# Attention and two-stage expert kernel: routing rounds, splits and first loads at other places

## The chip, the cores and the metric

The kernel runs on one core of a Trainium2 chip. The metric is the device time of one execution, in microseconds (us); lower is better. Names of engines: PE is TensorE (matmuls; PEld its weight loads), DVE is VectorE, ACT is ScalarE, POOL is GpSimd, and SP is SyncE, which here only issues DMAs.

## What is computed

```
# attention, 4 batches x 8 heads x 576 positions x 64
scores = q @ k.T / 8 + alibi bias, causal, window of 128; x = softmax(scores) @ v      -> x: 2304 x 512
# routing: every token gets one of 8 experts, 288 tokens each
logits = x @ w_gate                      # 2304 x 8
for idx in argsort(-logits.flatten()):   # greedy, best score first, until an expert is full
    tok, e = idx // 8, idx % 8; assign if tok is free and expert e has fewer than 288
for e in range(8):  y[mask_e] = relu(x[mask_e] @ w1[e]) @ w2[e]        # 512 -> 1024 -> 512
# dense layer
h = y @ w_in; out = (h * sigmoid(h)) @ w_out                            # 512 -> 2048 -> 512
```

## The kernel before

All work is written out by hand for each engine; semaphores order it, and every engine executes its list in order. There are two blocks.

**Attention.** 16 groups (batch, pair of heads) are worked through in 65 slots; group g's five row tiles (four of 128 rows, one of 64) are finished one after the other. When a group's tiles are normalised (DVE, `normalise`, L705), PE turns them (`turn_x`: four tiles into one PSUM bank, L410, the fifth into another, L413), DVE copies the first four to `xT` (`copy_x`, L626), ACT the fifth (`copy_x_end`, L551), and PE multiplies with the gate weights (`gate_logits`, L422, five matmuls, ten in the trace). For the last group nothing is left to run beside this.

**Routing of an expert.** The next expert to be filled, and its 288 tokens, are found by rounds of a search for a threshold. A round has an even part (PE counts, 20 small matmuls, L1102; DVE compares, `reached`, L1381) and an odd part (PE sums, L1106; DVE finds the digit and writes the next comparison matrix `test`). For expert 0, which is found before any expert runs, DVE writes `test` in two halves of 10 tiles (L1353, L1356), and PE counts the first (L1094) while DVE makes the second (L1102). For experts 1 to 7 it is one instruction (L1360). After the rounds come three closing parts: one in which the ranks are summed (L1109; before it the expert's number goes to SP, which may then load weights), one in which token numbers are collected (L1115; DVE then writes `tokens`, on which POOL's gather waits, and after some bookkeeping `out_tokens`), and one that updates the counts of free places (L1120, which waits for `out_tokens`). Expert j > 0 has 13 parts, numbered 0 to 12: rounds 0 to 9, ranks 10, tokens 11, counts 12. Expert 0 has 15.

**Experts.** Expert i is an A stage (expert i's two matrices, 16 slots) and an M stage (the dense layer for its batch, 32 slots): 48 slots in all. A slot is either `a` (12 matmuls into an `hp` bank; there are two) or `b` (12 matmuls in A, 6 or 9 in M, into `acc`). The order is a0, a1, a2, b0, a3, b1, a4, b2 and so on, so that b(f) runs two `a` slots behind a(f). Behind an M `a` slot ACT takes the sigmoid (`gate`, L1307), DVE multiplies (`h_raw`, L1561), ACT rounds (`h_h`, L1315) and POOL takes the rest (`h_l`, L1078). PE's a(f+2) reuses the bank of a(f) and so waits for `h_raw` of a(f), and b(f) waits for `h_l` of a(f).

All operands are split into a rounded and a remaining part. For a weight tile ACT makes the high part (L1256 for w1, L1261 for w2), DVE the low part of w1 (`low_a`, L1498), POOL that of w2 (`low_b`, L1064). Rings of four hold the tiles of each. For w of a new expert's first four tiles the splits stand at slots given by SPLIT_A and SPLIT_B, the loads in the order LOADS on SP's queue.

The parts of expert j's routing run inside expert j-1's 48 slots, at slots given by HOOK_LIST, after a set-up (SETUP_AT: `setup`, L1366 to the first `test`, some 15 DVE instructions). At a slot, the part comes ahead of the slot's own work, on PE as on DVE. The gather for expert j (`fetch`, three indirect DMAs of 96 rows, L1042) stands on POOL at the slot of part 11, and PE turns the gathered rows at slot 45 (X_AT).

For expert 0, SP issues eight weight loads (w1 and w2 tiles 0 to 3, alternating) as soon as the expert is known; POOL issues the gather a little later, then runs `low_b` for four tiles, while DVE waits for the gather to be issued (`fetch_sent`) and then runs `low_a`.

## Time and profile before

| | us |
|---|---|
| median of 3 runs | 894.79 |
| lowest and highest | 894.15, 895.1 |
| the profiled execution's own time | 896.79 |
| its span in the trace | 895.0 |
| PE busy | 846.1 (95%) |
| DVE, ACT, POOL busy | 503.9, 344.8, 290.1 |
| mean granted clock of PE | 0.975 |

The span is from the first to the last instruction; about 1.8 us lie around it. PE's busy time is modelled from pipelined matmuls, so small waits of PE can be hidden in it. In the text, a row `241.75 0.50 PE` means: begins 241.75 us after the span's start and takes 0.50 us.

### The profile page before, as it was taken

To read this page: it belongs to the slowest core of one execution; us is meant where nothing else is said; L and a number is where in the kernel's file an instruction comes from. 1 tells how busy PE (TensorE), PEld (TensorE's weight loads), DVE (VectorE), ACT (ScalarE), POOL (GpSimd) and SP (SyncE) were. 2 spreads that over 40 slices of the span, in tenths; PEclk is the share of its full clock that TensorE was granted. 3 is DMA by queue.
4 is the path that set the end of the run, shared out by engine and by line. 5 is a ranking of instruction groups with operands and counts; after the bars stand their busy time and mean duration, and the time that the engine had idled before them with its cause. 6 is when DMAs were issued, how large, how long until landed. Compare 5 with 4: busy or idle time off the path is not lost.

```text
span 895.0 us, 17483 instructions
## 1 busy us (share of the span) xinstructions
PE 846.1 (95%) x6605; PEld 790.2 (88%) x6605; DVE 503.9 (56%) x1618; ACT 344.8 (39%) x814; POOL 290.1 (32%) x306
## 2 busy tenths in 40 slices
PE   6999999962999999999999999999999999999998
PEld 6999999951998998899899889998998899899996
DVE  6667676757667386466628462666376466632111
ACT  4666666621333432433333233333332433433222
POOL 1333233413124422622432244225322522532223
PEclk9999999965899999999999999999999999999999
DMA  6666666414203121230412040403121240312000
GB/s 154 168 153 158 152 154 156 112 28 121 83 13 121 44 76 37 86 107 13 122 44 76 1 121 1 123 9 122 54 65 55 68 114 5 121 60 61 1 1 35
DMA packets 117252, 71.42 MB, mean 80 GB/s; under 512 B 61616, under 2 KB 103600, under 8 KB 117168
## 3 DMA queue, kind: packets, MB, share of 16 engines
q1 hardware_dynamic: 114192, 60.85, 25.2%
q0 software_dynamic: 2976, 9.44, 3.4%
q8 instruction: 53, 0.87, 0.4%
q14 instruction: 31, 0.25, 0.1%
HBM read 60.83 MB, written 9.44 MB: 79 GB/s over the span
## 4 chain that ended last, share of the span: by engine, by line
PE 65%; DVE 10%; DMA 2%; issue 1%; ACT 1%; POOL 1%; SPq 0%; POOLq 0%; DVEq 0%
PE hp L1148 11%; PE hp L1150 10%; PE hp L1149 10%; PE acc L1218 7%; PE acc L1220 7%; PE acc L1219 7%; PE acc L1148 4%; PE acc L1150 3%; PE acc L1149 3%; PE rt L1102 2%; DVE test L1360 2%; DVE h_raw L1561 1%; DMA rows<-x_rows,tokens 1%; DVE wa_l L1498 1%; DMA wa_raw<-in_moe_w_dram 1%
## 5 line engine op out<-in xcount | busy, mean ns | idle before, releaser
L1078 POOL TENSOR_TENSOR h_l<-h_raw,h_h 128x256 fp32r<-128x256 f32 (+1 forms) x128 | 103.6, 809 | 268.2 <-ACT h_h L1315 268.0
L1148 PE MATMUL hp<-xy_h,res_h 128*128 128x256 f32 (+1 forms) x512 | 154.6, 302 | 2.3 <-DVE h_raw L1561 2.3
L1561 DVE TENSOR_TENSOR h_raw<-hp,gate 128x256 f32<-128x256 f32 (+1 forms) x128 | 58.3, 456 | 171.1 <-ACT gate L1307 170.1
L1149 PE MATMUL hp<-xy_l,res_h 128*128 128x256 f32 (+1 forms) x512 | 151.4, 296 | 0.0
L1150 PE MATMUL hp<-xy_h,res_l 128*128 128x256 f32 (+1 forms) x512 | 151.3, 295 | 0.0
L1064 POOL TENSOR_TENSOR wb_l<-wb_raw,wb_h 128x512 fp32r<-128x512 f32 x64 | 86.5, 1353 | 139.6 <-ACT wb_h L1261 139.4
L1307 ACT ACTIVATE gate<-hp 128x256 f32<-128x256 f32 (+1 forms) x128 | 52.4, 409 | 171.0 <-PE hp L1150 170.0
L1218 PE MATMUL acc<-res_h,h_h 128*128 128x512 f32 x288 | 116.7, 405 | 0.0
L1220 PE MATMUL acc<-res_h,h_l 128*128 128x512 f32 x288 | 113.6, 395 | 0.0
L1219 PE MATMUL acc<-res_l,h_h 128*128 128x512 f32 x288 | 113.5, 394 | 0.0
L1148 PEld LDWEIGHTS hp<-xy_h,res_h 128*128 128x128 f32 x512 | 96.6, 189 | 8.5 <-DVE h_raw L1561 4.9
L1149 PEld LDWEIGHTS hp<-xy_l,res_h 128*128 128x128 f32 x512 | 96.4, 188 | 3.5
L1150 PEld LDWEIGHTS hp<-xy_h,res_l 128*128 128x128 f32 x512 | 96.5, 188 | 0.0
L1315 ACT ACTIVATE h_h<-h_raw 128x256 fp32r<-128x256 f32 (+1 forms) x128 | 56.9, 445 | 101.1 <-DVE h_raw L1561 101.1
L1148 PE MATMUL hp<-xy_h,wa_h 128*128 128x288 f32 x256 | 77.9, 304 | 0.6 <-DVE xy_l L1505 0.6
L1498 DVE TENSOR_TENSOR wa_l<-wa_raw,wa_h 128x512 fp32r<-128x512 f32 x64 | 60.3, 944 | 30.8 <-ACT wa_h L1256 26.8
L1149 PE MATMUL hp<-xy_l,wa_h 128*128 128x288 f32 x256 | 76.5, 299 | 0.0
L1150 PE MATMUL hp<-xy_h,wa_l 128*128 128x288 f32 x256 | 76.4, 299 | 0.0
L1148 PE MATMUL acc<-h_h,wb_h 128*128 128x288 f32 x256 | 76.3, 298 | 0.0
L1150 PE MATMUL acc<-h_h,wb_l 128*128 128x288 f32 x256 | 75.2, 294 | 0.0
L1149 PE MATMUL acc<-h_l,wb_h 128*128 128x288 f32 x256 | 75.2, 294 | 0.0
L480 PE MATMUL o_ps<-v_rows,pT 128*128 128x65 f32 x576 | 71.4, 269 | 0.0
(214 smaller groups left out, 1754.3 us busy)
## 6 DMA issues: line engine op xcount, KB each, us to landing
wa_raw<-in_moe_w_dram SPq DMA_DIRECT2D x64, 256.0 KB, 2.9
wb_raw<-in_moe_w_dram SPq DMA_DIRECT2D x64, 256.0 KB, 3.1
q_rows<-in_q_dram SPq DMA_DIRECT2D x32, 128.0 KB, 3.8
k_rows<-in_k_dram SPq DMA_DIRECT2D x32, 128.0 KB, 3.0
v_rows<-in_v_dram SPq DMA_DIRECT2D x32, 128.0 KB, 2.4
stage<-in_moe_w_in_dram SPq DMA_DIRECT2D x8, 512.0 KB, 4.5
x_rows<-x_rows_sb SPq DMA_DIRECT2D x16, 256.0 KB, 4.2
stage<-in_moe_w_out_dram SPq DMA_DIRECT2D x8, 512.0 KB, 4.6
```

Source lines behind the costliest of these rows:

```text
L480: last = nc.tensor.matmul(o_ps[s % 2][:, o:o + D + 1], weights, v_rows[g % RING_IN][:, kt, h, :], start=(i == 0), stop=(i == len(blocks) - 1))
L1064: pool.tensor_tensor(wb_l[w % RING][:], wb_raw[w % RING][:], wb_h[w % RING][:].bitcast(FP32), ALU.subtract).then_inc(wb_low, 1)
L1078: pool.tensor_tensor(h_l[:, cols], h_raw[:, cols], h_h[:, cols].bitcast(FP32), ALU.subtract).then_inc(g_low, 1)
L1148: nc.tensor.matmul(out_, weights_h, cols_h, start=start, stop=False)
L1149: nc.tensor.matmul(out_, weights_h, cols_l, start=False, stop=False)
L1150: return nc.tensor.matmul(out_, weights_l, cols_h, start=False, stop=stop)
L1218: nc.tensor.matmul(acc[t][:], h_h[:, m], res_h[:, o:o + DM], start=(b == 0), stop=False)
L1219: nc.tensor.matmul(acc[t][:], h_h[:, m], res_l[:, o:o + DM], start=False, stop=False)
L1220: last = nc.tensor.matmul(acc[t][:], h_l[:, m], res_h[:, o:o + DM], start=False, stop=(b == FT2 - 1))
L1315: nc.scalar.activation(h_h[:, h_cols(s, f)], h_raw[:, h_cols(s, f)], ACT.Copy).then_inc(g_high, 1)
L1498: nc.vector.tensor_tensor(wa_l[w % RING][:], wa_raw[w % RING][:], wa_h[w % RING][:].bitcast(FP32), ALU.subtract).then_inc(wa_low, 1)
L1561: nc.vector.tensor_tensor(h_raw[:, h_cols(s, f)], hp[(A_NO[s, f] - 1) % 2][:, 0:width], gate[:, 0:width], ALU.mult).then_inc(g_done, 1)
```

## The change

Five things are moved, and no arithmetic is added or taken away.

1. **Attention end.** For the last group, `turn_x` is cut in two: three tiles are turned ahead of the last weighted values (they are normalised by then), two behind them. Their logits are computed in the same two pieces. The copy of the three tiles goes from DVE to ACT (`copy_x_last`).
2. **Rounds of expert 0.** `test` is written as 14 and 6 tiles instead of 10 and 10.
3. **Slots of the parts** (counted in expert j-1's 48 slots):

| | set-up | parts 0 to 12 |
|---|---|---|
| before | 3 | 8, 9, 12, 13, 16, 17, 21, 22, 24, 25, 28, 31, 33 |
| after, j = 1 | 5 | 9, 10, 12, 13, 16, 20, 24, 25, 28, 29, 32, 35, 39 |
| after, j > 1 | 3 | 8, 9, 12, 13, 16, 20, 24, 25, 28, 29, 32, 35, 39 |

The loads of the next expert, which wait for part 9, go with it from slot 25 to 29, the gather with part 11 from 31 to 35.

4. **Splits of an expert's first four tiles** go from slots 31, 33, 35, 37 (`b` slots) to 38, 40, 42, 44 (`a` slots).
5. **First weights of expert 0.** SP issues w1 tiles 0 and 1, then waits until the gather is issued (`fetch_sent`), then w2 tile 0, w1 tile 2 and the rest. The splits of w2's four tiles and of w1's tile 3 go into the first slots of the A stage.

```diff
+SETUP_AT = {FIRST[2 * _j - 2] + (5 if _j == 1 else 3): _j for _j in range(1, E)}
+HOOK_LIST = {_j: [FIRST[2 * _j - 2] + _n for _n in ((9, 10, 12, 13) if _j == 1 else (8, 9, 12, 13))
+                  + (16, 20, 24, 25, 28, 29, 32, 35, 39)] for _j in range(1, E)}
...
+AHEAD = 14
+SECOND = 672
...
+LOADS = [("a", 0), ("a", 1), ("b", 0), ("a", 2), ("b", 1), ("a", 3), ("b", 2), ("b", 3)] + LOADS
+SPLIT_A, SPLIT_B = {0: [3]}, {0: [0], 1: [1], AT[0, "b", 0]: [2], AT[0, "b", 1]: [3]}
...
-        _n = max(FIRST[_s - 1] + 13, HOOK_LIST[_w // FT1][CLOSE[_w // FT1] - 1] + 6) + 2 * _f
+        _n = max(FIRST[_s - 1] + 13, HOOK_LIST[_w // FT1][CLOSE[_w // FT1] - 1] + 9) + 2 * _f
...
+                if (kind, w) == LOADS[2]:
+                    sp.wait_ge(fetch_sent, 1)
...
             fetch(0)
             pool.memset(mark[:], 0.0).then_inc(fetch_sent, 1)
-            for w in range(RING):
-                low_b(w)
...
-            for w in range(RING):
-                high_a(w)
-                high_b(w)
+            high_a(0)
+            high_a(1)
             for c in range(DC):
                 high_x(0, c, acc[c])
+            high_a(2)
...
+            turn_x_main(NG - 1)
             weighted_values(NS - 1)
-            turn_x(NG - 1)
-            gate_logits(NG - 1)
+            bank("e", NG - 1)
+            gate_logits(NG - 1, slice(0, main_tiles(NG - 1)))
+            turn_x_end(NG - 1)
+            gate_logits(NG - 1, slice(main_tiles(NG - 1), TB))
...
+            def copy_x_last(g):
+
+                n = TURN_NO["x", g]
+                w = P * main_tiles(g)
+                act.wait_ge(turned, n + 1)
+                act.wait_ge(lg_done, g)
+                nc.scalar.activation(xT[:, 0:w], m_ps[n % 2][:, 0:w], ACT.Copy).then_inc(x_taken, 1)
```

What this moves, as the engines' own lists show it. First PE at the end of attention (o_ps are the weighted values, m_ps<-x_rows_sb the turned tiles, m_ps<-wg,xT the logits); before:

```order
L458 MATMUL t_ps<-ident,p_even 128x2x64 x2
L480 MATMUL o_ps<-v_rows,pT 128x65 x8
L410 MATMUL m_ps<-ident,x_rows_sb 128x128 x4
L413 MATMUL m_ps<-ident,x_rows_sb 128x128
L422 MATMUL m_ps<-wg,xT 128x8 x5
```

And the same place on PE after the change:

```order
L479 MATMUL t_ps<-ident,p_even 128x2x64 x2
L501 MATMUL o_ps<-v_rows,pT 128x65 x4
L421 MATMUL m_ps<-ident,x_rows_sb 128x128 x3
L501 MATMUL o_ps<-v_rows,pT 128x65 x4
L442 MATMUL m_ps<-wg,xT 128x8 x3
L430 MATMUL m_ps<-ident,x_rows_sb 128x128 x2
L442 MATMUL m_ps<-wg,xT 128x8 x2
```

Three turned tiles and their logits now stand ahead of or beside the last values; two tiles and two logit matmuls are left behind them.

Next ACT at the start of the experts (wa_h and wb_h are high parts of w1 and w2 tiles, xy_h of the gathered rows, h_h the first results of the A stage); before:

```order
L1256 ACTIVATE wa_h<-wa_raw_3793 128x512
L1261 ACTIVATE wb_h<-wb_raw_3797 128x512
L1256 ACTIVATE wa_h<-wa_raw_3794 128x512
L1261 ACTIVATE wb_h<-wb_raw_3798 128x512
L1256 ACTIVATE wa_h<-wa_raw_3795 128x512
L1261 ACTIVATE wb_h<-wb_raw_3799 128x512
L1256 ACTIVATE wa_h<-wa_raw_3796 128x512
L1261 ACTIVATE wb_h<-wb_raw_3800 128x512
L1266 ACTIVATE xy_h<-acc 128x288 x4
L1301 ACTIVATE h_h<-hp 128x288 x2
```

The same place on ACT after the change:

```order
L1297 ACTIVATE wa_h<-wa_raw_3811 128x512
L1297 ACTIVATE wa_h<-wa_raw_3812 128x512
L1307 ACTIVATE xy_h<-acc 128x288 x4
L1297 ACTIVATE wa_h<-wa_raw_3813 128x512
L1342 ACTIVATE h_h<-hp 128x288
L1297 ACTIVATE wa_h<-wa_raw_3814 128x512
L1302 ACTIVATE wb_h<-wb_raw_3815 128x512
L1342 ACTIVATE h_h<-hp 128x288
L1297 ACTIVATE wa_h<-wa_raw_3811 128x512
L1302 ACTIVATE wb_h<-wb_raw_3816 128x512
```

Two weight tiles instead of eight stand ahead of the gathered rows; the others come behind the first results.

Last DVE in expert 0's M stage, between parts 11 and 12 of expert 1's routing (out_tokens ends part 11, spare is part 12, h_raw is an `a` slot's work, wa_l a split); before:

```order
L1479 TENSOR_TENSOR chosen<-chosen,tmp 128x20
L1463 SCALAR_TENSOR_TENSOR out_tokens<-rt,idx_low 32x1
L1463 SCALAR_TENSOR_TENSOR out_tokens<-rt,idx_low 32x2 x4
L1498 TENSOR_TENSOR wa_l<-wa_raw_3793,wa_h 128x512
L1561 TENSOR_TENSOR h_raw<-hp,gate 128x256
L1486 TENSOR_TENSOR spare<-spare,rt 128x8
L1487 TENSOR_SCALAR full<-spare 128x8
```

The same place on DVE after the change:

```order
L1518 TENSOR_TENSOR chosen<-chosen,tmp 128x20
L1502 SCALAR_TENSOR_TENSOR out_tokens<-rt,idx_low 32x1
L1502 SCALAR_TENSOR_TENSOR out_tokens<-rt,idx_low 32x2 x4
L1599 TENSOR_TENSOR h_raw<-hp,gate 128x256 x2
L1537 TENSOR_TENSOR wa_l<-wa_raw_3811,wa_h 128x512
L1525 TENSOR_TENSOR spare<-spare,rt 128x8
L1526 TENSOR_SCALAR full<-spare 128x8
```

Two `a` slots instead of one lie between the two parts, and the first split stands behind them.

## Rows read from the trace of the kernel before

**Rows 1.** The page: the granted TensorE clock in 40 slices, in tenths.

```profile
PEclk9999999965899999999999999999999999999999
```

**Rows 2.** Waits of PE, whole span: line, what ended them, us, times, longest.

```profile
PE acc L1235 <- DMA rows<-x_rows,tokens: 8.5, 1, 8.5
PE rt L1120 <- DVE out_tokens L1463: 8.1, 7, 1.3
...
PE hp L1148 <- DVE h_raw L1561: 2.3, 6, 0.4
```

**Rows 3.** Timeline, end of attention: start, us, engine, line, operation, [idle before].

```profile
186.97 0.28 DVE L705 TENSOR_TENSOR x_rows_sb<-o_ps,rden 64x128 f32<-64x128 f32 x1
...
187.40 0.92 PE L410 MATMUL m_ps<-ident,x_rows_sb 128*128 128x128 f32 x4 [0.86 <-DVE x_rows_sb L705]
...
188.57 0.28 ACT L551 ACTIVATE xT<-m_ps 128x128 f32<-128x128 f32 x1 [3.35 <-PE m_ps L413]
...
189.14 2.27 PE L422 MATMUL m_ps<-wg,xT 128*128 128x8 f32 x10 [0.61 <-DVE xT L626]
191.45 0.19 DVE L637 TENSOR_TENSOR logits<-m_ps,logits 128x32 f32<-128x32 f32 x1 [2.41 <-PE m_ps L422]
```

**Rows 4.** Timeline, one round of expert 0, DVE and PE.

```profile
198.70 0.65 DVE L1353 SCALAR_TENSOR_TENSOR test<-rungs,base,key_hi 128x410 bf16<-128x410 f32 x1
...
199.41 0.43 PE L1094 MATMUL rt<-choice,test 128*128 128x8 bf16 x10 [1.14 <-DVE test L1353]
199.96 0.43 PE L1102 MATMUL rt<-choice,test 128*128 128x8 bf16 x10
```

**Rows 5.** Timeline, from expert 0's first load to its first product.

```profile
212.15 0.41 SPq L998 DMA_DIRECT2D wa_raw<-in_moe_w_dram  x1
...
218.39 0.92 POOL L1042 DMA_INDIRECT rows<-x_rows,tokens  x1 [0.30 <-issue]
...
219.43 4.80 DVE L1498 TENSOR_TENSOR wa_l<-wa_raw,wa_h 128x512 fp32r<-128x512 f32 x2 [2.32 <-POOL mark L1068]
...
223.25 2.47 PE L1235 MATMUL acc<-ident,rows 96*128 96x96 f32 x12 [8.54 <-DMA rows<-x_rows,tokens]
...
226.33 0.58 PE L1148 MATMUL hp<-xy_h,wa_h 128*128 128x288 f32 x1 [0.60 <-DVE xy_l L1505]
```

**Rows 6.** All 24 gather DMAs (L1042): time from issue to landing.

```profile
DMA to landing us min/median/max: 3.0/3.1/6.0
```

**Rows 7.** Two stretches: busy PE, PEld, DVE, ACT, POOL, granted clock, DMA.

```profile
226.00:232.00 6.00, 5.67 (x24) 5.70 (x25) 3.41 (x11) 1.01 (x3) 0.00 (x0) 0.50 0.14 42
232.00:238.00 6.00, 6.00 (x47) 6.00 (x47) 4.65 (x15) 2.91 (x6) 0.00 (x0) 1.00 0.48 136
```

**Rows 8.** Timeline, parts 11 and 12 of expert 1, in expert 0's M stage.

```profile
279.96 0.66 PE L1115 MATMUL rt<-early,test 128*128 128x18 bf16 x20
...
283.91 0.80 DVE L1463 SCALAR_TENSOR_TENSOR out_tokens<-rt,idx_low 32x1 int32<-32x1 f32 x5
...
284.86 0.17 PE L1120 MATMUL rt<-row_counts,ones 128*128 128x8 bf16 x1 [1.32 <-DVE out_tokens L1463]
```

**Rows 9.** Timeline, part 5 of expert 1, and the PE wait behind it.

```profile
260.13 2.11 DVE L1360 SCALAR_TENSOR_TENSOR test<-rungs,base,key 128x1820 bf16<-128x1820 f32 x1
...
262.63 0.39 PE L1148 MATMUL hp<-xy_h,res_h 128*128 128x256 f32 x1 [0.38 <-DVE h_raw L1561]
```

**Rows 10.** Line L1360, the comparison matrices of experts 1 to 7: duration in ns.

```profile
L1360 DVE SCALAR_TENSOR_TENSOR test<-rungs,base,key_hi x21: 2114/3036/3041, 237.1 to 743.1; 128x1820 bf16<-128x1820 f32 x21
```

**Rows 11.** Timeline, DVE: the set-up of expert 1's routing begins.

```profile
234.72 0.32 DVE L1367 TENSOR_TENSOR liked<-logits,penalty 128x160 f32<-128x160 f32 x1
```

**Rows 12.** The chain that ended last: part 0 of expert 1 (start, us, what).

```profile
241.75 0.50 PE rt L1102 x20
```

**Rows 13.** Timeline, end of expert 0's M stage: its last h_l, and b15.

```profile
303.57 0.74 POOL L1078 TENSOR_TENSOR h_l<-h_raw,h_h 128x256 fp32r<-128x256 f32 x1 [2.10 <-ACT h_h L1315]
...
305.82 0.40 PE L1218 MATMUL acc<-res_h,h_h 128*128 128x512 f32 x1
```

More of the change, by code:

```diff
@@ L141 @@
 RING_NEG = 3
-LG = P
 def slot_units(s):
@@ L596, in _ @@
                     copy_q_low(g + 1)
+            copy_x_last(NG - 1)
             copy_x_end(NG - 1)
@@ L633, in add_logits @@
                     dve.wait_ge(lg_added, g)
-                part = m_ps[TURN_NO["e", g] % 2][:, LG:LG + E * TB].rearrange("p (t e) -> p t e", e=E)
+                o = logits_at(g)
+                part = m_ps[TURN_NO["e", g] % 2][:, o:o + E * TB].rearrange("p (t e) -> p t e", e=E)
                 main = logits[:, TB * b:TB * b + TB - 1, :]
@@ L829, in load_key @@
     return max(AT[s, kind, f], HOOK_LIST[w // FT1][CLOSE[w // FT1] - 1] if w >= FT1 else 0)
-LOADS = sorted([(kind, w) for w in range(E * FT1) for kind in "ab"], key=lambda load: load_key(*load))
-SPLIT_A, SPLIT_B = {}, {}
+LOADS = sorted([(kind, w) for w in range(RING, E * FT1) for kind in "ab"], key=lambda load: load_key(*load))
+LOADS = [("a", 0), ("a", 1), ("b", 0), ("a", 2), ("b", 1), ("a", 3), ("b", 2), ("b", 3)] + LOADS
+SPLIT_A, SPLIT_B = {0: [3]}, {0: [0], 1: [1], AT[0, "b", 0]: [2], AT[0, "b", 1]: [3]}
 for _w in range(RING, E * FT1):
@@ L898, in experts @@
         at_least = test[:, 0:NT * KW[1]].rearrange("p (t k) -> p t k", k=KW[1])
-        halves = [test[:, o:o + KW[0] * NT // 2].rearrange("p (t k) -> p t k", k=KW[0]) for o in (0, SECOND)]
+        pieces = [test[:, o:o + KW[0] * n].rearrange("p (t k) -> p t k", k=KW[0])
+                  for o, n in ((0, AHEAD), (SECOND, NT - AHEAD))]
         onehot = test[:, 0:NT * BLOCK].rearrange("p (t k) -> p t k", k=BLOCK)
@@ L1092, in part @@
                     pe.wait_ge(half_part, h // 2)
-                    for t in range(NT // 2):
+                    for t in range(AHEAD):
                         nc.tensor.matmul(rt[:, 0:E], test[:, KW[0] * t:KW[0] * t + P], choice[:, t, :],
@@ L1098, in part @@
                 if h < CLOSE[j] and h % 2 == 0:
-                    for t in range(NT // 2 if j == 0 and h > 0 else 0, NT):
-                        o = KW[j] * t if j > 0 or h == 0 else SECOND + KW[0] * (t - NT // 2)
+                    for t in range(AHEAD if j == 0 and h > 0 else 0, NT):
+                        o = KW[j] * t if j > 0 or h == 0 else SECOND + KW[0] * (t - AHEAD)
                         last = nc.tensor.matmul(rt[:, 0:E], thresholds[:, o:o + P], choice[:, t, :],
@@ L1351, in try_thresholds @@
                 if j == 0:
-                    t = NT // 2
-                    nc.vector.scalar_tensor_tensor(halves[0], rung[:, None, :].to_broadcast([P, t, k]),
-                                                   base[:, 0:1], keys[:, 0:t, None].to_broadcast([P, t, k]),
-                                                   ALU.add, ALU.is_le).then_inc(half_part, 1)
-                    nc.vector.scalar_tensor_tensor(halves[1], rung[:, None, :].to_broadcast([P, t, k]),
-                                                   base[:, 0:1], keys[:, t:NT, None].to_broadcast([P, t, k]),
-                                                   ALU.add, ALU.is_le).then_inc(dve_part, 1)
+                    for piece, tiles, made in ((pieces[0], slice(0, AHEAD), half_part), (pieces[1], slice(AHEAD, NT), dve_part)):
+                        n = tiles.stop - tiles.start
+                        nc.vector.scalar_tensor_tensor(piece, rung[:, None, :].to_broadcast([P, n, k]), base[:, 0:1],
+                                                       keys[:, tiles, None].to_broadcast([P, n, k]),
+                                                       ALU.add, ALU.is_le).then_inc(made, 1)
                     return
@@ L1539, in _ @@
             low_a(2)
-            low_a(3)
             after(0, HOOKS[0] - 1)
```

51 lines of the change are left out of this document (30 added, 21 removed).

## The prediction

> **What bounds the kernel now.** I read the page first, then the waits of PE, then the timeline at each wait. PE is the bound in attention and in the experts. Between them lies a stretch from about 187 to 226 us in which nothing but expert 0's routing and gather is left, and PE is mostly idle; there the clock granted to PE is down, too [rows 1]. So the time is the length of that stretch plus PE's work, plus the few places where PE waits inside the experts. Those waits are short to list: 8.5 us for expert 0's gathered rows, 8.1 us in seven waits of part 12 for `out_tokens`, 2.3 us in six waits for `h_raw` [rows 2]. The change goes for all three, and for the ends of the stretch.
>
> **Attention end.** Now, from the end of the last normalisation (186.97 + 0.28 = 187.25) to the first added logits at 191.45 are 4.2 us: five turned tiles, two copies, ten logit matmuls at 2.27 / 10, some 0.21 us apart [rows 3]. After the change two tiles, one copy and four matmuls remain. Six matmuls less are 1.3 us. Three turned tiles less are about 0.5 us, since four of them take 0.92 with their latency. The copy on the path is now the one that ends just before 189.14; with 256 columns on ACT it should be near 0.4 (128 columns take 0.28), which gains 0.3. Against that, three turned tiles come ahead of the last weighted values and delay the last normalisation, by 0.4 us, and PE still has the six early logit matmuls beside it, about 0.1 us more. Sum: 1.3 + 0.5 + 0.3 - 0.5 = 1.6 us gained. The ends are 1.2 (more delay ahead) and 2.0 (the clock falls later and the four matmuls run faster). The last rows of x are stored to memory beside this; their DMAs are issued right after the normalisation, so they move back by the same 0.4 us only, and 6 us of ranking lie behind them.
>
> **Rounds of expert 0.** PE counts its first ten tiles 0.71 us after DVE begins the first half, starts on the second ten 1.26 after it, and needs 0.43 for them [rows 4]. DVE's two instructions together have the same length at 14 and 6 tiles. The first takes 4/10 of 0.43 longer, 0.17, so PE starts at 0.88, and 14 matmuls at 0.027 apart ((0.43 - 0.17) / 9, 0.17 being the length of one alone, as in [rows 8]) are issued by 1.26, just when the second part is ready. Then six instead of ten remain: 4 x 0.027 = 0.11 us. Five such rounds: 0.5 us, and not below 0.2.
>
> **Gather of expert 0.** SP's eight loads start at 212.15, ahead of the gather, whose last DMA is issued at 218.39 [rows 5]. The 24 gather DMAs of the kernel land 3.0 to 6.0 us after issue, with a median of 3.1 [rows 6]; expert 0's are the only ones that share the DMA engines with eight fresh weight loads, and PE gets their rows from 223.25 on, turning all twelve pieces in one go. After the change only two loads (0.5 MB) are ahead. They should be in before the first gather moves data, since they lose six rivals. The last gather then lands at 218.39 + 3.1 = 221.5; all pieces of the first two DMAs are turned by then. What follows is one piece (about 0.3), ACT's high part and DVE's low part (0.4 and 0.5) and their hand-overs: first product at about 223.0 against 226.33, so 3.3 us gained. DVE must have `low_a` of tiles 0 and 1 done, which now takes 4.80 us from 219.43 [rows 5] because POOL runs `low_b` at the same time; with `low_b` moved behind, it is over well before 222. Held from both sides: if the loads that now start at 219.4 still disturb the last gather, the gain is 2.3; with nothing left beside it, 3.6. The clock is at its lower level, 1.2 GHz, for the first 5.7 us of products and at 2.4 GHz from 232.0 on [rows 7]. I take it that this stretch moves along unchanged. The late tiles: w1's tile 2 is wanted 5.7 us after the first product (228.7), and is loaded near 223.5; w2's tile 0 one slot, 1.5 us, later. Both have several us in hand, tile 3 and the other w2 tiles about two.
>
> **Part 12.** PE's part 11 ends at 279.96 + 0.66 = 280.6, `out_tokens` at 283.91 + 0.80 = 284.7, and part 12 follows at 284.86; PE has only one `b` and one `a` slot in between, 284.86 - 1.32 - 280.6 = 2.9 us, and waits 1.32 us [rows 8]. So an M slot is 1.4 us. With four slots in between PE has 5.7 us, while DVE's chain stays 4.1 us: the wait goes altogether, in all seven experts. That is 8.1 us [rows 2]. What is late next is `h_raw` of the `a` at slot 36, which DVE begins near 284.8; the `a` at slot 40 wants its bank, five slots behind part 11, at 280.6 + 7.0 = 287.6. So nothing takes the wait's place. POOL issues three gather DMAs there, about 3.5 us during which no `h_l` is made; `b` runs two `a` slots behind, with 5.7 us between a(f) and b(f), so this is covered.
>
> **Part 5.** DVE makes the key and a 2.11 us comparison matrix in this part, so that `h_raw` is late and PE stands still at 262.63 [rows 9]. Part 5 stands ahead of a1, where no `b` slot separates a1 and a2. At slot 20 it stands ahead of a3; between a3 and the a5 that needs its bank lie b1, a4 and b2, 4.3 us instead of the 2.9 of a2 and b0. The wait goes: 2.3 us by the wait view; matmul ends are modelled and hide part of each wait, so I take 3.0, with 2.3 and 4.5 as ends.
>
> The other parts keep at least three slots behind an odd one, 4.2 us against a longest matrix of 3.04 us [rows 10]; they cost and gain nothing. The same instructions run, so PE's own work is unchanged.
>
> **Moved splits.** On an `a` slot ACT now makes two high parts (about 1.3 us) between the sigmoid and `h_h`, so `h_l` comes some 0.8 us later. The tightest place is the end of the M stage: `h_l` of a15 ends at 303.57 + 0.74 = 304.3, and b15, which waits for it, begins at 305.82 [rows 13]. 1.5 us in hand against 0.8: no wait.
>
> **First A stage of expert 0.** Here the change adds to a busy place. DVE's set-up begins at 234.72, and part 0 is at 241.75 [rows 11, 12]; set-up and part 0 go back by two slots and one, so a slot of room is lost (12 products at 6.00 / 47 us, 1.5 us [rows 7]), and POOL now has four more `low_b` at the same time. A matrix takes 2.11 us undisturbed and 3.04 mostly [rows 10]; that is 0.9 us more for each `low_b` it meets. Behind the set-up come `low_a` and `h_l`, on which a6 waits. I put 0.5 us on it, between 0 and 2.5.
>
> The Trainium skill says in "GPSIMD Engine Reference", section Specifications, that GpSimd shares its SBUF interfaces with VectorE, and that they get in each other's way where a VectorE instruction has two SBUF inputs. By that rule nearly each of the set-up's instructions waits while POOL works, and not only the matrix. The 4.80 us for two low parts [rows 5] agree. Taken strictly, the set-up would be longer by all of POOL's added work that falls into it, and the time would be the first rival's.
>
> **Sum.** 1.6 + 0.5 + 3.3 + 8.1 + 3.0 - 0.5 = 16.0 us. The profiled execution took 896.8 us, so it would take 880.8. The median of the runs is 2.0 us lower, 894.8, and gives **878.8 us**. The best ends of the terms together give 2.0 + 0.5 + 3.6 + 8.1 + 4.5 = 18.7, or 876.1.
>
> **Rivals.** (1) *DVE and POOL collide in the first A stage.* If DVE loses 0.9 us for each of three `low_b`, `reached` of part 0 and `h_l` of a4 come after PE wants them, and 2.5 us are lost instead of 0.5: 880.8. For it speaks the lost slot; against it that part 0 had some 2 us in hand. (2) *The gather doesn't gain.* Its DMAs are slow for another reason than the loads, the expert's first products come where they came: 3.3 us less, 882.1. Against it: 3.1 us in the other gathers, with loads just ended. (3) *The waits come back elsewhere.* DVE has the same work in each expert, and a later `h_raw` or split takes about 1 us in each of seven: 878.8 + 7 = 885.8. Against it: DVE is busy for 503.9 of 895.0 us only. (4) *Slower.* The loads and splits now end next to the turn of the next expert's rows at slot 45. If POOL's last `low_b` and ACT's high parts push `h_l` of a15 and the high parts of the new rows behind b15 and the next a0, PE waits there in each expert. The point at which this decides is 16.0 / 7 = 2.3 us in each; it needs a delay of 1.5 + 2.3 = 3.8 us where I find 0.8. If two splits (ACT 1.3, DVE 0.7, POOL 1.3 us each) piled up, 4.5 us of delay, the loss would be 3.0 us in each, 21 in all: 899.8.
>
> **How the numbers follow.** Forecast 0.62, rival 1 0.14, rival 2 0.09, rival 3 0.09, rival 4 0.04, and 0.02 for a change that does nothing by the clock. The range 876.0 to 884.5 holds the forecast with its bounds, rivals 1 and 2, and leaves out 3 and 4. About 0.2% of the time, 1.8 us, is what a measurement can tell from no change. Faster: forecast and rivals 1 to 3, 0.94; the same 0.02; slower 0.04.
>
> **What would show it.** Right: no wait of `row_counts` matmuls for `out_tokens`, none of PE for `h_raw` behind part 5, gather landings of 3.1 us for expert 0, the first product 5.4 us earlier on the span's clock (1.6 + 0.5 + 3.3), two low parts of w1 near 1.4 us together. Wrong: a new wait of PE for `reached`, `test` or `h_l` in the first A stage (rival 1), landings still near 6 us (rival 2), waits of a b15 or a0 for `h_l` or `xy_l` at the end of the M stages (rivals 3 and 4).

## The result, and the profile after

The changed kernel takes **882.28 us**, the median of four runs (880.27 to 882.73), against 894.68 of the kernel before (894.15 to 895.1, four runs). The ratio is 0.9857 with a 95% interval from 0.984 to 0.9874. It is faster, by 12.4 us; the forecast was 878.8 us, so its time lies within the range on record and 3.5 us above the number. All medians here leave out two executions that took far longer than the rest, one of e9 (1048 us) and one of the kernel before beside it (4694 us).

The profiled execution of the changed kernel took 882.7 us, with a span of 881.0 us; that of before took 896.8 with a span of 895.0. On the traces the gain is 14.0 us. First the waits of PE over the whole span (line, what ended them, us in total, times, longest), which answer to [rows 2]:

```profile
PE acc L1276 <- DMA rows<-x_rows,tokens: 5.3, 3, 4.4
PE rt L1147 <- DVE reached L1420: 4.5, 8, 2.2
...
PE rt L1143 <- DVE test L1399: 0.3, 1, 0.3
```

The waits for `out_tokens` and for `h_raw`, 8.1 and 2.3 us before, are not in the list any more. The wait for the gathered rows fell from 8.5 to 5.3 us. And there are two new things: PE waits 0.3 us for a matrix (`test`), and, before, no wait for `reached` (the small tensor between a round's counts and its sum) was above 0.7 us, now one takes 2.2.

The end of attention, in the timeline (start, us, engine, line, operation, [idle before]), answers to [rows 3]:

```profile
187.89 0.28 DVE L741 TENSOR_TENSOR x_rows_sb<-o_ps,rden 64x128 f32<-64x128 f32 x1
...
188.31 0.41 PE L430 MATMUL m_ps<-ident,x_rows_sb 128*128 128x128 f32 x2 [0.22 <-DVE x_rows_sb L741]
...
188.76 0.38 ACT L577 ACTIVATE xT<-m_ps 128x256 f32<-128x256 f32 x1 [1.62 <-PE m_ps L430]
...
189.29 0.58 PE L442 MATMUL m_ps<-wg,xT 128*128 128x8 f32 x4 [0.56 <-ACT xT L577]
189.91 0.19 DVE L673 TENSOR_TENSOR logits<-m_ps,logits 128x32 f32<-128x32 f32 x1 [1.74 <-PE m_ps L442]
```

Two tiles, one copy, four matmuls. The logits are added 189.91 - 188.17 = 1.74 us after the last normalisation, 4.2 before. The four matmuls are some 0.11 us apart, not 0.21. To compare the two executions, take a point that the change doesn't touch, the last turn of probabilities on PE; before, and then after:

```profile
184.38 0.42 PE L458 MATMUL t_ps<-ident,p_even 128*128 128x128 f32 x2
185.02 0.41 PE L479 MATMUL t_ps<-ident,p_even 128*128 128x128 f32 x2
```

The execution of the changed kernel is already 0.64 us behind there. From this point to the added logits are 7.07 us before and 4.89 after, so the attention end itself gives 2.2 us. The gather of expert 0 and what follows it answers to [rows 5]:

```profile
210.07 1.03 SPq L1041 DMA_DIRECT2D wa_raw<-in_moe_w_dram  x2
...
211.93 0.70 PE L1156 MATMUL rt<-early,test 128*128 128x18 bf16 x20 [2.87 <-DVE early L1495]
...
216.32 0.92 POOL L1085 DMA_INDIRECT rows<-x_rows,tokens  x1 [0.31 <-issue]
...
217.35 0.34 SPq L1047 DMA_DIRECT2D wb_raw<-in_moe_w_dram  x1
217.36 1.29 DVE L1537 TENSOR_TENSOR wa_l<-wa_raw,wa_h 128x512 fp32r<-128x512 f32 x2 [2.33 <-POOL mark L1111]
...
219.77 0.90 PE L1276 MATMUL acc<-ident,rows 96*128 96x96 f32 x4 [0.68 <-DMA rows<-x_rows,tokens]
...
221.28 0.58 PE L1189 MATMUL hp<-xy_h,wa_h 128*128 128x288 f32 x1 [0.60 <-DVE xy_l L1544]
```

The rows of the last gather DMA, issued at 216.32, are turned from 219.77 on, 3.45 us later; the two low parts of w1 (`wa_l`) take 1.29 us, where they took 4.80. From the tokens (211.93) to the first product (221.28) are 9.35 us; before they were 12.32.

Up to here the kernel does what the forecast said. What follows the first product does not. This is DVE in expert 0's A stage, from the start of expert 1's set-up to part 1, and POOL beside it:

```profile
232.65 0.32 DVE L1406 TENSOR_TENSOR liked<-logits,penalty 128x160 f32<-128x160 f32 x1
...
233.36 1.46 DVE L61 TENSOR_TENSOR liked<-liked,best 128x160 f32<-128x160 f32 x1
...
236.18 2.11 DVE L1399 SCALAR_TENSOR_TENSOR test<-rungs,base,key_hi 128x1820 bf16<-128x1820 f32 x1
238.22 1.25 DVE L83 TENSOR_SCALAR half<-bits 128x20 int32<-128x20 int32 x1
239.50 1.22 DVE L84 TENSOR_SCALAR key_lo<-half 128x20 f32<-128x20 int32 x1
...
242.70 0.15 DVE L1420 TENSOR_TENSOR reached<-rt,left 91x8 bf16<-91x8 f32 x1
```

```profile
233.35 1.29 POOL L1107 TENSOR_TENSOR wb_l<-wb_raw,wb_h 128x512 fp32r<-128x512 f32 x1 [0.87 <-ACT wb_h L1302]
236.51 4.18 POOL L1107 TENSOR_TENSOR wb_l<-wb_raw,wb_h 128x512 fp32r<-128x512 f32 x2 [1.87 <-ACT wb_h L1302]
```

Three instructions of the set-up that take 0.32, 0.17 and 0.18 us in the kernel before take 1.46, 1.25 and 1.22 here, each beside a low part of w2 on POOL. The set-up lasts from 232.65 to 240.7, 8.1 us; before, 4.8, from 234.72 to 239.53, where this line ends:

```profile
239.35 0.18 DVE L84 TENSOR_SCALAR key_lo<-half 128x20 f32<-128x20 int32 x1
```

Behind the set-up stand `wa_l` and `h_l`, and `reached` of part 0 comes at 242.7. PE, in the same place:

```profile
242.91 0.18 PE L1147 MATMUL rt<-reached,ones 128*128 128x8 bf16 x1 [2.21 <-DVE reached L1420]
```

And three stretches there (length; busy PE, PEld, DVE, ACT, POOL with counts; granted clock; DMA share; GB/s):

```profile
236.00:240.00 4.00, 3.75 (x44) 3.52 (x44) 3.93 (x5) 1.36 (x3) 3.49 (x2) 1.00 0.23 66
240.00:243.00 3.00, 0.80 (x7) 0.56 (x6) 2.82 (x6) 0.00 (x0) 0.69 (x1) 1.00 0.28 87
243.00:247.00 4.00, 4.00 (x20) 4.00 (x21) 2.90 (x4) 0.93 (x2) 0.21 (x1) 0.57 0.00 1
```

PE stands for 2.2 us and goes on at 242.91, and then the granted clock is at 1.2 GHz for most of 243 to 247: 20 matmuls instead of 47 or so. 4.00 x (1 - 0.57) = 1.7 us are lost to that. The spell is too short for the clock line of the page, where the slice from 242 to 264 us stays at 9. What that line shows against [rows 1] is the 8 in the ninth slice, where a 6 was: at the end of attention the clock falls later.

```profile
PEclk9999999985899999999999999999999999999999
```

**Where the time went.** I take the stages from first product to first product on PE. All values are us of the two profiled executions.

| stretch | before | after | change | forecast |
|---|---|---|---|---|
| start to expert 0's logits added | 191.45 | 189.91 | -1.54 | -1.6 |
| logits added to tokens | 22.56 | 22.02 | -0.54 | -0.5 |
| tokens to first product | 12.32 | 9.35 | -2.97 | -3.3 |
| expert 0, A stage | 29.87 | 34.07 | +4.20 | +0.5 |
| M stages of experts 0 to 6, summed | 376.45 | 363.43 | -13.02 | -11.1 |
| all else | | | -0.2 | 0 |
| span | 895.0 | 881.0 | -14.0 | -16.0 |

One by one the M stages of experts 0 to 6 went from 51.02, 50.75, 50.74, 71.36, 51.04, 50.78 and 50.76 us to 48.91, 48.63, 48.92, 70.50, 48.92, 48.63 and 48.92. (Expert 3's M stage has 384 rows, the other six have 256.)

### The profile page after: what moved, and what is told of

Same layout as the page of the kernel before. It is cut to its first block, busy times and chain, and to the rows that moved or that the text cites. A ratio compares the mean times of both kernels' runs of the same rounds, so it can differ in the third digit from the quotient of the medians.

```text
span 881.0 us, 17486 instructions
## 1 busy us (share of the span) xinstructions
PE 843.8 (96%) x6605; PEld 790.5 (90%) x6605; DVE 491.4 (56%) x1617; ACT 343.2 (39%) x815; POOL 300.2 (34%) x306
## 4 chain that ended last, share of the span: by engine, by line
PE 72%; DVE 4%; POOL 1%; DMA 1%; issue 1%; ACT 0%; SPq 0%; POOLq 0%; DVEq 0%
PE hp L1189 12%; PE hp L1190 11%; PE hp L1191 11%; PE acc L1259 8%; PE acc L1261 8%; PE acc L1260 7%; PE acc L1189 4%; PE acc L1191 3%; PE acc L1190 3%; PE rt L1143 2%; DVE wa_l L1537 1%; PE rt L1156 0%; DVE test L1399 0%; DVE test L1395 0%; DMA rows<-x_rows,tokens 0%
## 5 line engine op out<-in xcount | busy, mean ns | idle before, releaser
L1119 POOL TENSOR_TENSOR h_l<-h_raw,h_h 128x256 fp32r<-128x256 f32 (+1 forms) x128 | 115.7, 904 | 263.5 <-ACT h_h L1356 263.4
L501 PEld LDWEIGHTS o_ps<-v_rows,pT 128*128 128x128 f32 x576 | 69.4, 192 | 0.0
```

What stands on the lines that cost most here:

```text
L501: last = nc.tensor.matmul(o_ps[s % 2][:, o:o + D + 1], weights, v_rows[g % RING_IN][:, kt, h, :], start=(i == 0), stop=(i == len(blocks) - 1))
L1119: pool.tensor_tensor(h_l[:, cols], h_raw[:, cols], h_h[:, cols].bitcast(FP32), ALU.subtract).then_inc(g_low, 1)
```

## The experiments

The kernels ran in groups that share runs of the kernel before on one chip; its median was 895.71 us beside e1 to e4, 894.91 beside e5 to e8 and 895.76 beside e9 to e11, so that ratios compare across groups and medians only to about 1 us. Two theories of the A stage stood against each other after the result: **POOL's low parts** beside the set-up lengthen it (the first rival's mechanism), or the set-up simply begins two slots too late. The forecast's terms were tried one by one as well.

### e1: the slots alone

The kernel before with the new slots of set-up, parts and splits, nothing else.

```diff
-SETUP_AT = {FIRST[2 * _j - 2] + 3: _j for _j in range(1, E)}
-HOOK_LIST = {_j: [FIRST[2 * _j - 2] + _n for _n in (8, 9, 12, 13, 16, 17, 21, 22, 24, 25, 28, 31, 33)]
-             for _j in range(1, E)}
+SETUP_AT = {FIRST[2 * _j - 2] + (5 if _j == 1 else 3): _j for _j in range(1, E)}
+HOOK_LIST = {_j: [FIRST[2 * _j - 2] + _n for _n in ((9, 10, 12, 13) if _j == 1 else (8, 9, 12, 13))
+                  + (16, 20, 24, 25, 28, 29, 32, 35, 39)] for _j in range(1, E)}
...
-        _n = max(FIRST[_s - 1] + 13, HOOK_LIST[_w // FT1][CLOSE[_w // FT1] - 1] + 6) + 2 * _f
+        _n = max(FIRST[_s - 1] + 13, HOOK_LIST[_w // FT1][CLOSE[_w // FT1] - 1] + 9) + 2 * _f
```

> The kernel before with the new slots of set-up, parts and splits alone; first weights, attention end and halves as before. Theory 1 (the loss in expert 0's A stage comes from POOL's four added low parts, which hold DVE's set-up): A stage 0 stays near 29.9 us (up to 31), M stages give back 13.0 us as in the changed kernel, 882 to 883 in all. Theory 2 (it comes from the set-up standing two slots later): A stage 0 is near 34 us, and the time near 886.

Measured: 884.49 us against 895.71, ratio 0.9872 (0.9857 to 0.9888), as far above the expected range as below the rival's 886, so that the A stage has to decide. The seven M stages are as in the changed kernel to 0.03 us, so the whole 13.0 us of them come from the slots. The A stage takes 30.74 us, 0.9 more than before, with one wait of 1.2 us for `reached`; in the stretch of the wait the granted clock stays up (columns as above):

```profile
PE rt L1106 <- DVE reached L1381: 3.5, 8, 1.2
```

```profile
244.00:248.00 4.00, 2.80 (x22) 2.57 (x21) 3.66 (x7) 0.00 (x0) 1.07 (x1) 1.00 0.27 66
```

The 0.9 is too small a price, though, because the clock came up sooner in this execution. The first 5.64 us from the first product on ran at a mean granted clock of 0.50 in the kernel before (226.33 to 231.97), and here at

```profile
226.28:231.92 5.64, 5.64 (x28) 5.64 (x28) 3.09 (x10) 0.89 (x3) 0.00 (x0) 0.61 0.15 45
```

which gives back 5.64 x 0.11 = 0.6 us. So the later set-up alone costs about 1.5 us, not 4.2.

### e2: the first loads alone

The kernel before with the last part of the change: two loads ahead of the gather, six behind it, high and low parts of w2 spread over the first slots.

```diff
-LOADS = sorted([(kind, w) for w in range(E * FT1) for kind in "ab"], key=lambda load: load_key(*load))
-SPLIT_A, SPLIT_B = {}, {}
+LOADS = sorted([(kind, w) for w in range(RING, E * FT1) for kind in "ab"], key=lambda load: load_key(*load))
+LOADS = [("a", 0), ("a", 1), ("b", 0), ("a", 2), ("b", 1), ("a", 3), ("b", 2), ("b", 3)] + LOADS
+SPLIT_A, SPLIT_B = {0: [3]}, {0: [0], 1: [1], AT[0, "b", 0]: [2], AT[0, "b", 1]: [3]}
...
+                if (kind, w) == LOADS[2]:
+                    sp.wait_ge(fetch_sent, 1)
...
```

> The kernel before with the first weights alone moved behind the gather (loads, high and low parts); set-up at slot 3, parts at 8, 9. Theory 1 (POOL's added work): A stage 0 is longer than 29.9 us by 1 to 4, which eats the 3.0 us that the gather gives: 892.5 to 895.5. Theory 2 (later set-up): A stage 0 stays at 29.9 and the time is 894.7 - 3.0 = 891.7.

Measured: 896.64 us, ratio 1.0013 (1.0004 to 1.0022), 1.1 us above the expected range. The gather gains as it does in the changed kernel: from the tokens (213.96) to the first product (223.22) are 9.26 us instead of 12.32, 3.06 less. The A stage then takes 33.25 us instead of 29.87, 3.4 more. Its wait, and the stretch with the fall of the clock:

```profile
PE hp L1149 <- DVE h_l L1555: 1.7, 1, 1.7
```

```profile
240.00:244.00 4.00, 3.20 (x17) 3.06 (x18) 2.72 (x7) 0.79 (x2) 0.00 (x0) 0.73 0.13 50
```

The set-up is at its old slot here, and still PE waits 1.7 us and the clock falls behind it. This part of the change gains nothing by itself, and is rather a loss, of 0.4 to 2.0 us: what the gather gives, the A stage takes back.

### e3 and e4: the set-up back at its old slot

The changed kernel with expert 1's set-up at slot 3 again. In e3 parts 0 and 1 stay at 9 and 10, in e4 they are at 8 and 9. The edit of e3:

```diff
-SETUP_AT = {FIRST[2 * _j - 2] + (5 if _j == 1 else 3): _j for _j in range(1, E)}
+SETUP_AT = {FIRST[2 * _j - 2] + 3: _j for _j in range(1, E)}
```

> The changed kernel with expert 1's set-up back at slot 3, its parts left at 9, 10, 12, 13. Theory 2 (later set-up; two slots are 3.1 us of room, and 2.3 us of wait were seen): no wait of PE in A stage 0, no fall of the clock behind it, A stage 0 near 29.9 us, 882.3 - 4.2 = 878.1. Theory 1: the set-up meets POOL's low parts of slots 1 to 3 instead, and a wait of 0.5 to 2 us stays: 879 to 881.5.

> The changed kernel with set-up, part 0 and part 1 of expert 1 as before, at 3, 8, 9. One slot (1.5 us) less of room for the set-up than in the run with parts at 9. If room alone decides: the set-up with POOL in its way takes up to 8 us (8.1 in the changed kernel), slots 3 to 8 last 8.3, so the wait is under 1 us: 878.1 to 879.5. If the clock falls only behind a wait of some 2 us, it stays up here.

Measured: e3 882.08 us, ratio 0.9847 (0.9834 to 0.9861); e4 881.39 us, ratio 0.9842 (0.9828 to 0.9855), against 0.9857 (0.984 to 0.9874) for the changed kernel, which the runs can't tell apart. The A stages take 33.97 and 33.45 us, against 34.07. The wait only moves to another tensor. Of e3, and then of e4 with its clock:

```profile
PE hp L1189 <- DVE h_l L1593: 3.0, 1, 3.0
```

```profile
PE hp L1189 <- DVE h_l L1593: 1.8, 1, 1.8
```

```profile
236.00:240.00 4.00, 2.28 (x9) 2.28 (x10) 3.24 (x8) 0.00 (x0) 0.33 (x1) 0.71 0.17 52
```

In e4 another wait, of 0.6 us for a matrix, ends 0.7 us ahead of this one. The theory of the late set-up falls: with the slots of before, the stage is still 3.6 us longer than before. Of e4's expectation, "room alone decides" falls too, and so does the clock staying up behind a wait under 2 us.

### e5 and e6: two low parts of w2 at another time

If POOL's work is the cause, it has to go where DVE has nothing long to do. In both kernels ACT makes the high parts of w2's tiles 0 and 1 right behind that of w1's tile 2, and POOL their low parts ahead of its loop; tiles 2 and 3 take the slots that 0 and 1 had. e5 also has the set-up at 3 and the parts at 8 and 9, e6 keeps 5, 9 and 10.

```diff
-SPLIT_A, SPLIT_B = {0: [3]}, {0: [0], 1: [1], AT[0, "b", 0]: [2], AT[0, "b", 1]: [3]}
+SPLIT_A, SPLIT_B = {0: [3]}, {0: [2], 1: [3]}
...
             pool.memset(mark[:], 0.0).then_inc(fetch_sent, 1)
+            low_b(0)
+            low_b(1)
...
             high_a(2)
+            high_b(0)
+            high_b(1)
```

> The changed kernel with expert 1's set-up and parts back at 3, 8, 9, and the first four w2 tiles split sooner: tiles 0 and 1 ahead of slot 0, tiles 2 and 3 in slots 0 and 1 (they land by 224.3, before the first relu). Theory 1 (each low part of POOL that falls into the set-up costs DVE 1.1 us, and the clock falls behind the wait this makes): POOL is done by about 229, the set-up lasts 4.8 instead of 8.6 us, PE doesn't wait, the clock stays up, A stage 0 is 29.5 to 30, first product unchanged: 881.4 - 3.8 = 877.6. Rival (DVE simply has too much to do in this stage once low parts come late): A stage 0 stays above 32, 880 and more.

> The changed kernel with only the four w2 splits sooner (tiles 0, 1 ahead of slot 0, tiles 2, 3 in slots 0, 1); set-up at 5, parts at 9, 10 as in the changed kernel. Theory 1: what is left is what the slots alone cost, A stage 0 near 30.7 (a wait of 1.2 us for reached, no fall of the clock): 882.2 - 3.3 = 878.9. Rival: 882.

Measured: e5 **877.54 us** (876.85 to 877.93) against 894.91, ratio 0.9804 (0.9791 to 0.9817); e6 877.99 us, ratio 0.9812 (0.9798 to 0.9825). The A stage takes 29.46 us in e5, less than before the change, and 31.19 in e6. In e5 PE waits nowhere in it. The set-up's instructions on DVE and the stretches on PE:

```profile
229.79 0.33 DVE L61 TENSOR_TENSOR liked<-liked,best 128x160 f32<-128x160 f32 x1
...
233.51 0.17 DVE L83 TENSOR_SCALAR half<-bits 128x20 int32<-128x20 int32 x1
233.71 0.18 DVE L84 TENSOR_SCALAR key_lo<-half 128x20 f32<-128x20 int32 x1
```

```profile
236.00:240.00 4.00, 4.00 (x31) 3.93 (x32) 3.16 (x6) 0.93 (x2) 2.04 (x2) 1.00 0.23 66
```

The same instructions are at 0.33, 0.17 and 0.18 us again, since no low part runs on POOL between 229.2 and 235.5. In e6, with the late slots, PE waits for `reached` once, and the clock stays up:

```profile
241.52 0.18 PE L1149 MATMUL rt<-reached,ones 128*128 128x8 bf16 x1 [1.20 <-DVE reached L1424]
```

```profile
240.00:244.00 4.00, 2.80 (x22) 2.57 (x21) 3.65 (x6) 0.53 (x2) 0.47 (x1) 1.00 0.22 66
```

Between e5 and e6 the A stage differs by 1.7 us. Some 0.3 of it is again the clock at the start of the stage (a mean of 0.58 over the first 5.64 us in e5, 0.52 in e6), so the later slots cost some 1.4 us here, as in e1. The medians differ only by 0.45, which their runs can't tell apart; by the traces the later slots are a loss, by the runs they are no gain, and no more.

### e7: all eight loads ahead of the gather again

The changed kernel without the wait of SP, so that POOL's low parts stay where the change put them and only the loads move.

```diff
-                if (kind, w) == LOADS[2]:
-                    sp.wait_ge(fetch_sent, 1)
```

> The changed kernel without SP's wait: all eight first loads are issued ahead of the gather again, the w2 splits stay in the A stage. Theory A (the loads slow the gather): its last rows land some 6 us after issue instead of 3.4, low_a stays at 0.65 us each, first product 2.7 us later. Theory B (POOL's and DVE's splits set the first product): it comes at the changed kernel's time.

Measured: 885.03 us, ratio 0.9884 (0.9868 to 0.9899). The slowest gather DMA, and the first turn, product and low parts:

```profile
DMA to landing us min/median/max: 3.0/3.1/8.0
```

```profile
217.32 1.29 DVE L1535 TENSOR_TENSOR wa_l<-wa_raw,wa_h 128x512 fp32r<-128x512 f32 x2 [2.32 <-POOL mark L1109]
...
221.71 2.18 PE L1274 MATMUL acc<-ident,rows 96*128 96x96 f32 x12 [9.10 <-DMA rows<-x_rows,tokens]
...
224.49 0.58 PE L1187 MATMUL hp<-xy_h,wa_h 128*128 128x288 f32 x1 [0.60 <-DVE xy_l L1542]
```

The first gather DMA of expert 0 now takes the longest, from 213.65 to 221.7; all three land within a microsecond of each other. (In e1 and e8, which leave the first loads as before, they take 5.0 to 7.9 us; in the kernel before the trace has only the third's, 6.0.) The tokens are at 211.90, so the first product comes 12.59 us behind them, 3.2 more than with the wait. `wa_l` stays short. The two causes of the forecast's gather term are apart: the loads delay the rows, POOL's low parts stretch `wa_l`, and it is the delayed rows that PE waits for. The A stage behind is as long as in the changed kernel, 34.16 us, with the same wait of 2.2 us.

### e8: the attention end and the rounds alone

The kernel before with the tile-by-tile end of attention and the halves of 14 and 6 tiles.

```diff
-            weighted_values(NS - 1)
-            turn_x(NG - 1)
-            gate_logits(NG - 1)
+            turn_x_main(NG - 1)
+            weighted_values(NS - 1)
+            bank("e", NG - 1)
+            gate_logits(NG - 1, slice(0, main_tiles(NG - 1)))
+            turn_x_end(NG - 1)
+            gate_logits(NG - 1, slice(main_tiles(NG - 1), TB))
...
-SECOND = 512
+
+AHEAD = 14
+SECOND = 672
...
```

> The kernel before with the attention end and the 14 and 6 halves alone. From the traces the attention end gives 1.5 to 2.2 us (logits 1.55 us earlier, with the last values 0.6 us later in that execution) and the halves 0.5: first product 2.0 to 2.7 us earlier, stages unchanged, 893.0 to 893.7 beside a before of 895.7.

Measured: 893.01 us over 11 runs, ratio 0.9979 (0.997 to 0.9988): 1.9 us, with 1.1 and 2.7 as ends, for 1.6 + 0.5 = 2.1 forecast. The A stage is 29.36 us long (29.87 before) and the M stages sum to 376.0 (376.45).

### e9, e10, e11: one slot table entry back at a time

All three start from e5, where the A stage doesn't disturb. e9 puts part 5 back from 20 to 17, e10 part 12 from 39 to 37 (two slots behind part 11, as before the change), e11 the splits of the next expert's first tiles from 9 to 6 slots behind.

```diff
-                  + (16, 20, 24, 25, 28, 29, 32, 35, 39)] for _j in range(1, E)}
+                  + (16, 17, 24, 25, 28, 29, 32, 35, 39)] for _j in range(1, E)}
```

```diff
-                  + (16, 20, 24, 25, 28, 29, 32, 35, 39)] for _j in range(1, E)}
+                  + (16, 20, 24, 25, 28, 29, 32, 35, 37)] for _j in range(1, E)}
```

```diff
-        _n = max(FIRST[_s - 1] + 13, HOOK_LIST[_w // FT1][CLOSE[_w // FT1] - 1] + 9) + 2 * _f
+        _n = max(FIRST[_s - 1] + 13, HOOK_LIST[_w // FT1][CLOSE[_w // FT1] - 1] + 6) + 2 * _f
```

> The best kernel so far (early w2 splits, set-up and parts at 3, 8, 9) with part 5 back at slot 17, the other parts as in the changed kernel. Forecast's term: PE waits for h_raw again, 0.5 us in each of six M stages of 256 rows, 3 us in all: 880.6. Rival (part 5's place gives more than the wait that a view shows, since all M stages gained 13.0 us where the waits sum up to 11.6): up to 4.5 us, 882.

> The same best kernel with part 12 at slot 37, two slots behind part 11 as before. Forecast's term: a wait of 1.3 us for out_tokens in each of seven M stages, 8.1 us in all: 885.7. Rival: POOL's low part no longer stands beside DVE's bookkeeping (it moved to slot 38), so DVE's chain is 0.7 us shorter and the wait comes back at 0.6 us only: 882.

> The same best kernel with the next expert's first splits at slots 35, 37, 39, 41 instead of 38, 40, 42, 44. If the place of the splits gives nothing by itself once part 12 is late: the same time, 877.5. If low parts beside DVE's bookkeeping still cost PE something: M stages longer by 0.2 to 1 us each, 879 to 884.

| kernel | us (against 895.76) | ratio, 95% | M stages 0 to 6, us more than in e5 | sum |
|---|---|---|---|---|
| e9, part 5 at 17 | 881.28 | 0.9839 (0.9817 to 0.986) | 0.65, 0.66, 0.64, 0.02, 0.66, 0.70, 0.65 | 4.0 |
| e10, part 12 at 37 | 880.85 | 0.9836 (0.9819 to 0.9854) | 0.66, 0.69, 0.40, 0.00, 0.68, 0.72, 0.41 | 3.6 |
| e11, splits 3 slots earlier | 880.01 | 0.9828 (0.981 to 0.9845) | 0.42, 0.54, 0.35, 0.02, 0.44, 0.60, 0.35 | 2.7 |

By the ratios against e5's 0.9804 the three cost 3.1, 2.9 and 2.1 us, a little less than the stages say and within what four runs each can tell. Each entry gives its own wait of PE, of e9, e10 and e11 in this order:

```profile
PE hp L1191 <- DVE h_raw L1603: 2.3, 6, 0.4
```

```profile
PE rt L1163 <- DVE out_tokens L1506: 1.9, 4, 0.6
```

```profile
PE hp L1185 <- DVE h_raw L1603: 1.3, 4, 0.4
```

The first is the wait of before to the tenth. The second is not: `out_tokens` costs at most 0.6 us where it cost 1.3 at the same distance in slots. What shortened it is one instruction of the bookkeeping between part 11's counts and `out_tokens`, first in e11 with the early splits, then in e10 with the late ones (e5 has the same 0.17):

```profile
280.98 0.95 DVE L1522 TENSOR_TENSOR chosen<-chosen,tmp 128x20 f32<-128x20 f32 x1
```

```profile
281.73 0.17 DVE L1522 TENSOR_TENSOR chosen<-chosen,tmp 128x20 f32<-128x20 f32 x1
```

With the early splits a low part on POOL runs from 280.60 to 281.89 and ends with this instruction. The kernel before had the same there. So the moved splits took 0.8 us off DVE's chain to `out_tokens`, and part 12 at its old distance waits 0.6 instead of 1.3 us.

The third wait is new: PE's turn of the next expert's rows (L1185) waits for `h_raw`. It doesn't come from `chosen`, which is as long (0.87 us) in expert 3's M stage, where e11 loses nothing. It comes from an instruction of part 12 on 128x8 elements, ahead of `h_raw` in DVE's list:

```profile
286.14 3.36 DVE L1530 TENSOR_SCALAR full<-spare 128x8 f32<-128x8 f32 x1
286.21 1.32 POOL L1107 TENSOR_TENSOR wb_l<-wb_raw,wb_h 128x512 fp32r<-128x512 f32 x1
287.46 0.75 POOL L1121 TENSOR_TENSOR h_l<-h_raw,h_h 128x256 fp32r<-128x256 f32 x1
288.15 1.30 POOL L1107 TENSOR_TENSOR wb_l<-wb_raw,wb_h 128x512 fp32r<-128x512 f32 x1
```

POOL has three instructions in a row there, as they piled up behind the gather's DMAs, and DVE's is through only behind the third. `full` takes 3.4 to 3.6 us in just the six M stages that lose 0.35 to 0.60 us, and 0.17 in expert 3's and in the seven of e5. In the kernel before it took at most 0.34: this pile-up belongs to e11's own mix of early splits and a late part 12.

## Why the prediction was right, and where it was off

**Attention end** (forecast 1.6, 1.2 to 2.0). By the span's clock the logits are added 1.54 us earlier, but the changed kernel's execution was 0.64 us behind at a point ahead of the change; the end itself gives 2.2 us, a little more than the best end. So that 1.54 met 1.6 is luck. The ten traces with the new end all have 4.9 us from that point to the logits, the three with the old one 7.1 to 7.2. e8 with the rounds gives 1.9 of 2.1 forecast, with 2.7 as its upper end. The forecast's second end, faster matmuls because the clock falls later, is what happened: four at 0.11 us, not 0.21. The other side is that the last normalisation ends 0.9 us later (188.17 against 187.25); 0.64 of it is the execution, and 0.3 the work put ahead of it (I had put 0.4).

**Rounds** (0.5): 0.54. Right.

**Gather** (3.3, 2.3 to 3.6): 2.97 in the changed kernel, 3.06 in e2, 3.2 in e7. Right in mechanism, and rival 2 falls. The last gather DMA took 3.4 us to its landing instead of 3.1. The loads behind it begin at 217.35 while it is under way, which is the likely cause but isn't shown: over all traces with late loads it took 3.2 to 3.6 us. It is the bound I had given, met a third of the way.

**Part 12, part 5 and the moved splits** (8.1 + 3.0 + 0 = 11.1): 13.0, of which each M stage but expert 3's has 1.8 to 2.2. All waits named are gone and none came back, so rivals 3 and 4 fall. e9 measures the part 5 term alone at 4.0, where 3.0 was taken and 4.5 was the end. A wait that the view puts at 2.3 us thus cost 4.0; that modelled matmul ends hide the rest is the likely reading. The failing step is *Moved splits: no wait*. I asked only whether they would cost something at their new place, and not what they cost at the old one, where a low part on POOL stretched DVE's chain from part 11 to part 12 by 0.8 us. In e10 part 12 stands as close to part 11 as before, and the M stages are still 376.45 - 366.95 = 9.5 us shorter than before; less the 4.0 of part 5, 5.5 us are left for the splits and for parts 6 to 11, which moved too. One at a time the three entries give 4.0 + 3.6 + 2.7 = 10.3 of the 13.0. Where the other 2.7 belongs stays open: it may be lost only when two entries are back together, or come with parts 6 to 11, which no run puts back. So the 8.1 us of part 12 were not its own alone, and the sum came near because the splits' share was in it.

**First A stage** (-0.5, from 0 to -2.5): -4.2. This is the term that was mis-sized, and the forecast's largest error. Its direction and its mechanism were on record, as the first rival, whose size of 2.5 was too small as well. Three steps failed in it.

First, the price of a low part. I charged 0.9 us for each one met, from the matrix that takes 3.04 instead of 2.11 us. The rows show that any instruction can be the one that waits, a 128x20 one too, and that it waits until POOL is through: `L61` begins at 233.36 and ends at 234.8, POOL's low part runs from 233.35 to 234.64. Beside the matrix it is the other way round: POOL's two low parts from 236.51 take 4.18 us, not 2.6, since the first gets going only when the matrix, 236.18 to 238.29, is done; then it holds `L83`, and the second holds `L84`. Three low parts cost DVE 1.14 + 1.08 + 1.04 = 3.3 us, the whole difference between 8.1 and 4.8.

The Trainium skill says in "GPSIMD Engine Reference", section Specifications, that GpSimd and VectorE share SBUF interfaces and contend where VectorE's instruction has two SBUF inputs or is in a 2-port mode. The trace agrees that they contend, and by more than I let it: the prediction had given this rule its strict reading, all of POOL's added work on the set-up, and taken the milder one. `L83` and `L84`, with one tensor as input, are held like `L61`, with two; whether they ran in a 2-port mode no trace shows. So the prediction's "nearly each of the set-up's instructions" doesn't follow from two inputs alone, as some six of them have only one.

Second, the cover. I had some 2 us in hand for part 0 and charged the lost slot little. e1 and e6 give the slot its price: a wait of 1.2 us with the set-up short, and 1.4 to 1.5 us on the stage. With 3.3 us more on DVE the wait is 2.2. e3 and e4 show that another slot helps by 0.6 us at most, and e5, where the low parts go and the stage is 29.46 us with no wait, that POOL's work is the cause.

Third, the clock. A wait of PE was charged with its length. Here the clock fell behind it, and 1.7 us more were lost. 2.2 for the wait, 1.7 for the clock, and 0.3 for another wait for a matrix (`test`, L1399) come to the 4.2. The fit is a little better than it should be: the clock also came up 0.4 us sooner after the first product than before (5.2 us against 5.6), which hides 0.2 us. The prediction took it that this stretch moves along unchanged; over all traces it is 3.8 to 5.6 us long.

**The base.** 14.0 us on the traces became 12.4 us between the medians. The profiled execution of before was 2.0 us above its median, that of after 0.45 above its own. I had taken 2.0 off for both. Of the 3.5 us between forecast and result, 2.0 are thus the terms (3.7 too little for the A stage and 0.4 for what lies ahead of it, less 1.9 for the M stages and 0.2 for all else, which gained more than forecast), and 1.5 the base. (With the 0.64 us taken out by which the changed kernel's execution was behind ahead of the change, it is 1.3 and 2.2.) The A stage and the M stages both lie outside their bounds, on opposite sides; that the sum is near is in part luck. Of the base, the granted clock explains a part: the executions of before beside the experiments are of two kinds, at a mean of 0.974 to 0.976 or of 0.978, with medians 0.5 to 0.7 us apart, and the profiled one has 0.975. Why it lies still higher stays open.

**What is left of the change.** The gather's 3 us were given back in the A stage in full, as e2 shows. The better kernel is e5: the change without the later set-up, and with w2's first two low parts taken between the gather and the loop. It takes 877.54 us, 17.4 less than the kernel before beside it, where the changed kernel gained 12.4.

## What to carry to other kernels

Where two engines hold each other up, look at the longest serial chain of the one that the matmuls wait for, and put the other's work where no such chain runs; a chain of many short instructions is no safer than one long one. When work is moved, price its old place as well as its new one: here the splits gave back microseconds that a look at the new place alone could not find. Look at the other engine's list, too, for instructions that pile up: three of them in a row held one small instruction for 3.4 us. And charge a wait of PE with the clock behind it once it is long: in this kernel a wait of 1.2 us cost 1.4 to 1.5, and one of 2.2 cost 3.9.
